# Noise values in the token rows, two weight halves moved, and a new order of output products in a two-layer mixture-of-experts kernel

## The reference

```python
# first mixture: 3072 x 8 logits, greedy from the largest, cap = 384 tokens per expert
logits = x @ w_gate
for e in range(E):
    h = np.maximum(x[assigned == e] @ w1[e], 0.0)
    out[assigned == e] = h @ w2[e]
# second mixture, on the first one's output
logits = x @ w_gate
noise_scale = np.log1p(np.exp(x @ w_noise))
noisy_logits = logits + noise_scale * noise        # noise: one row of 8 values per token
top2 = np.argpartition(-noisy_logits, 2, axis=1)[:, :2]
...                                                # softmax over the two, sum of both experts
```

## Time and profile before

| | us |
|---|---|
| median of 3 runs (1318.83 to 1322.05) | 1318.96 |
| profiled execution, device time | 1320.37 |
| its span, first to last instruction | 1318.5 |
| TensorE busy | 1231.4 (93%) |
| VectorE busy | 914.4 (69%) |
| ScalarE busy | 572.1 (43%) |
| GpSimd busy | 286.2 (22%) |

### The profile page before, as it was taken

How to read it: one execution, slowest core, us unless ns; L and a number is a source line. 1 busy time by engine, 2 the same in 40 slices (tenths; PEclk the granted TensorE clock), 3 DMA queues, 4 the chain that set the end, 5 groups by cost and what they waited for, 6 DMA issues and landing times.

```text
span 1318.5 us, 27799 instructions
## 1 busy us (share of the span) xinstructions
PE 1231.4 (93%) x9680; PEld 1096.5 (83%) x9680; DVE 914.4 (69%) x1818; ACT 572.1 (43%) x1224; POOL 286.2 (22%) x346
## 2 busy tenths in 40 slices
PE   7999983299999999999999999999999999999997
PEld 6888872278787787888898999989999898999986
DVE  4777765887887888765696666666666666766662
ACT  4666650123333233344415544544455444544541
POOL 4000000202202102120213323324233242333322
PEclk9999995589999999999999999999999999999999
DMA  7878744433332432543315233233333423334210
GB/s 146 169 169 163 166 97 182 153 113 109 125 120 70 147 133 65 194 147 107 110 34 192 72 107 111 81 104 106 126 123 120 144 79 104 100 125 135 88 43 13
DMA packets 174298, 154.65 MB, mean 117 GB/s; under 512 B 105117, under 2 KB 137885, under 8 KB 174240
## 3 DMA queue, kind: packets, MB, share of 16 engines
q1 hardware_dynamic: 151552, 102.83, 27.8%
q0 software_dynamic: 16128, 44.56, 11.0%
q10 hardware_dynamic: 6560, 6.49, 1.4%
HBM read 206.13 MB, written 33.75 MB: 182 GB/s over the span
## 4 chain that ended last, share of the span: by engine, by line
PE 38%; issue 37%; DVE 10%; POOL 9%; DMA 3%; ACT 1%; POOLq 1%; DVEq 0%; SPq 0%; ACTq 0%
PE bank L789 8%; PE bank L769 8%; DMA out<-result,token_now 3%; PE bank L645 3%; POOL partial L421 3%; POOL out L431 3%; PE bank L654 2%; PE bank L633 2%; POOL held L401 2%; PE bank L1001 2%; PE bank L669 2%; POOL x L405 2%; PE bank L715 2%; PE bank L1028 2%; PE bank L754 1%
## 5 line engine op out<-in xcount | busy, mean ns | idle before, releaser
L572 DVE TENSOR_TENSOR w_part<-w_sb,w_part 128x1024 fp32r<-128x1024 f32 x280 | 341.7, 1224 | 97.1 <-ACT w_part L566 89.1
L566 ACT CAST w_part<-w_sb 128x1024 fp32r<-128x1024 f32 x280 | 290.6, 1046 | 205.1 <-PE bank L1028 152.2
L1001 PEld LDWEIGHTS bank<-x2T,w_part 128*128 128x128 f32 x2688 | 326.3, 192 | 4.6 <-DVE x2T L1558 1.6
L1001 PE MATMUL bank<-x2T,w_part 128*128 128x256 f32 x2688 | 327.9, 283 | 1.8 <-DVE x2T L1558 1.8
L1028 PE MATMUL bank<-w_part,h2T 128*128 128x512 f32 x1344 | 312.6, 391 | 0.0
L1028 PEld LDWEIGHTS bank<-w_part,h2T 128*128 128x128 f32 x1344 | 250.2, 188 | 51.0
L789 PE MATMUL bank<-w_part,hT 128*128 128x512 f32 x576 | 156.5, 409 | 3.7 <-DVE w_part L572 3.7
L769 PE MATMUL bank<-xgT,w_part 128*128 128x384 f32 x768 | 146.5, 344 | 0.9 <-DVE xgT L1222 0.9
L1913 ACT ACTIVATE h2T<-bank 128x512 fp32r<-128x512 f32 x112 | 66.9, 598 | 180.4 <-PE bank L1001 141.3
L379 POOL DMA_INDIRECT xg<-x_dram,token_of x24 | 29.6, 1232 | 507.0 <-DVE token_of L1258 266.0
L769 PEld LDWEIGHTS bank<-xgT,w_part 128*128 128x128 f32 x768 | 133.6, 191 | 2.9 <-DVE xgT L1222 1.4
(11 more groups left out here) (281 smaller groups left out, 1306.2 us busy)
## 6 DMA issues: line engine op xcount, KB each, us to landing
w_sb<-in_moe_w SPq DMA_DIRECT2D x280, 512.0 KB
k_in<-in_k SPq DMA_DIRECT2D x32, 240.0 KB
v_in<-in_v SPq DMA_DIRECT2D x32, 240.0 KB
q_in<-in_q SPq DMA_DIRECT2D x32, 192.0 KB
x_dram<-x_sb SPq DMA_DIRECT2D x32, 192.0 KB, 3.1
out<-zeros SPq DMA_DIRECT2D x1, 6144.0 KB, 19.7
y_dram<-y_sb ACTq DMA_DIRECT2D x24, 256.0 KB, 2.0
x<-y_dram,slot_now POOLq DMA_INDIRECT x56
```

Of the source, the lines that this page charges most:

```text
L566: scalar.copy(split_part(0, c), raw_part(c)).then_inc(hi_ready[c], 1)
L572: nc.vector.tensor_tensor(split_part(1, c), raw_part(c), split_part(0, c).bitcast(F32), ALU.subtract).then_inc(lo_ready[c], 1)
L1001: last = nc.tensor.matmul(bank[2 + g % 2][:, at:at + TILE], w1_part[a][:, kt, f * P:(f + 1) * P], x2T[b][:, kt, :], start=(f % 2 == 0 and ...
```

## The change

Three things change.

1. `x_dram` gets rows of 520 values: 512 of x and the token's 8 noise values. ScalarE's queue issues one copy of the whole noise array into the last 8 columns, after the attention has stored x. The gather of a token row brings its noise along, and a new ScalarE instruction, `copy_noise`, copies it to `noise_g` behind `xg_high(k, 2)`. The 24 noise gathers go. GpSimd's first gather waits for the copy (`noise_stored`), the later ones for `copy_noise` of the expert before.
2. Low halves move in VectorE's `step`: w1's last quarter (c = 3) from digit 6 to digit 5, between `met` and `delta`; w2's first quarter (c = 4) from behind `chosen` to digit 6; w2's second (c = 5) from the end of the step to behind `chosen`. ScalarE's high halves of c = 4 and 5 move with them.
3. The 24 products are done in the order 0 to 5, 8, 9, 6, 7, 10 to 23, in all bodies, and `before_votes[2]` goes from 9 to 10.

```diff
@@ TensorE
+            order = tuple(range(6)) + (8, 9, 6, 7) + tuple(range(10, TPE * FT))
             def combine(e, a, b):
-                for i in range(a, b):
+                for i in order[a:b]:
...
-                before_votes = (0, 6, 9, 12, 15, 20, 22)
+                before_votes = (0, 6, 10, 12, 15, 20, 22)
@@ VectorE, step, per digit s
                         if s >= 3:
-                            w_low(k, s - 3, 1)
+                            w_low(k, s - 3 if s < 6 else CH, 1)
                     dve.wait_ge(counts_up, n * len(SHIFTS) + s + 1)
...
+                        if s == 5:
+                            w_low(k, 3, 1)
                         if s == 6:
                             xg_low(k, 1)
@@ VectorE, step, behind the digits
                     xg_low(k, 2)
-                    w_low(k, CH, 1)
+                    w_low(k, CH + 1, 1)
...
                 if k is not None:
-                    w_low(k, CH + 1, 1)
                     s1_low(k, 3)
@@ ScalarE, step
                     xg_high(k, 0)
+                    w_high(k, CH, 1)
...
                     xg_high(k, 2)
-                    w_high(k, CH, 1)
+                    copy_noise(k)
+                    w_high(k, CH + 1, 1)
...
                     s1_high(k, 0)
-                    w_high(k, CH + 1, 1)
                     s1_high(k, 1)
@@ ScalarE, new
+            def copy_noise(e):
+                nc.scalar.copy(noise_g[:, bass.ds(e * TPE, TPE), :], xg[:, :, DM:DM + E]).then_inc(noise_in, 1)
...
+            act.dma_start(x_dram[:, DM:DM + E], moe2_noise[:, :]).then_inc(noise_stored, 16)
@@ GpSimd
                     pool.wait_ge(xg_turned, e * TPE)
+                    pool.wait_ge(noise_in, e)
+                else:
+                    pool.wait_ge(noise_stored, 16)
...
-                for c in range(e * TPE, (e + 1) * TPE):
-                    pool.indirect_dma_start(out=noise_g[:, c, :], out_offset=None, in_=moe2_noise[:, :],
```

## The result

Eight runs of each kernel on the same chip gave 1323.49 us for the changed kernel (1322.73 to 1324.66) and 1319.56 for the kernel before: ratio 1.0027, 95% interval [1.0018, 1.0036]. The change costs 3.6 us by the ratio and 3.9 by the medians, where my sum had 2.1. The profiled execution took 1323.39 us with a span of 1321.6 (before 1320.37 and 1318.5).

A forecast was written before the change was run, and what follows sets the result against it. The prediction took the hand-overs between TensorE and VectorE in the expert loop as the bound. Its terms, 1.05 - 0.6 + 0.25 + 0.5 + 0.9 = +2.1 us, gave 1321.1 us on the median 1318.96; range 1314.9 to 1323.8.

The forecast's parts named there:

- Products 8 and 9 ahead: Five loop steps: TensorE's 0.76 us wait turns into other waits, each step ends 0.21 us later; +1.05 us.
- the three waits I named: TensorE's new waits in the loop: for `above` of digits 2 and 3 and for `met` of digit 3.
- The eighth step: Step of experts seven and eight: a later `copy_y` delays ScalarE's queue and TensorE's third transpose by 0.87 us; +0.9 us.
- ScalarE's copy: Loop: the new noise copy on ScalarE makes the low half, tally and tie flags 0.1 us later; +0.5 us.
- The low half at the end of the step: w2's second quarter leaves the place before the last `s1_low`: gain 0.12 us a step, -0.6 us over five.
- The inserted low half: w1's last quarter between `met` and `delta` of digit 5: cover suffices by 0.11 us; +0.25 us over five steps.
- The rival in which it is paid: The half inserted at digit 5 delays TensorE by 0.55 us a step, giving 1323.8 us; chance 0.10.
- The noise: Noise gathers leave GpSimd, one copy into token rows is through before the first gather: 0 us, bounds 0 and +1.
- The waits simply vanish: Rival: TensorE's 0.76 and 0.58 us waits per loop step are gained whole, 6.6 us, giving 1312.4; chance 0.12.
- half of them: Rival: the 0.24 us lead is kept and the 0.58 us gained, -4.1 us, giving 1314.9; chance 0.04.
- The noise gathers cause the odd wait: Rival: they cause VectorE's 2.06 us idle before `met` of digit 5; without them 0.25 us return, 1320.8; chance 0.09.
- The port rule: Skill's rule that two-SBUF-input VectorE and SBUF-reading GpSimd instructions block each other; low half would lose up to 1 us.

The follow-up runs named there:

- e2_order: The kernel before with only the new product order (8 and 9 ahead of 6 and 7): 1320.65 us, ratio 1.0011.
- e4_noise: The kernel before with all noise edits of the change, but the old product order and weight halves: 1322.23 us, ratio 1.0022.
- e1_pad96: The kernel before with rows of xg 96 bytes a partition wider, so the buffers behind it begin 96 bytes later: 1322.37 us, ratio 1.0020.
- e3_halves: The kernel before with only the moved weight halves, noise still gathered by GpSimd: 1319.92 us, ratio 1.0005.
- e12_fill_halves: e11_fill with the moved weight halves of the change added: 1313.90 us, ratio 0.9957 to the kernel before.
- e13_place96: The kernel before with xg's rows unchanged and 96 unused bytes a partition behind them, moving the later buffers: ratio 1.0018.
- e9_one_ahead: The kernel before with only product 8 ahead of 6 and 7 in the loop's steps and fillings redistributed: 1315.94 us, ratio 0.9971.
- e0_again: The kernel before, unchanged, run and profiled a second time: 1318.79 us, ratio 1.0000.
- e11_fill: The kernel before with loop fillings moved to TensorE's waits: product 0, products 8 and 9, and the last gate product earlier: 1314.25 us, ratio 0.9961.
- e8_pad64: The kernel before with 64 unused bytes a partition behind xg, moving the later buffers by 64 bytes: ratio 1.0017.

## Why the prediction was right, and where not

**Products 8 and 9 ahead (+1.05).** Right, place by place: e2_order has +0.22 a step against my 0.21. Of the three waits I named two are there, 0.47 us before the count of s2 (I said 0.6) and 0.43 for `met` of s3. The 0.1 to 0.2 us before the count of s3 don't show.

**The eighth step (+0.9).** Right: +0.96 in e2_order, and the chain `copy_y`, high half, low half, `xg_low`, third transpose is the one forecast.

**ScalarE's copy (+0.5).** Right, path and size: 0.10 us a step between e4_noise and e1_pad96, by way of the low half and the tie flags.

**The low half at the end of the step (-0.6).** Its size was wrong: 0.0 us in e3_halves. I had taken off what `s1_low` waits for ScalarE and kept 0.12 us, and had not followed it beyond the count of s0. In the changed kernel the count of s0 does come 0.18 us sooner, but from it to the vote of s1 it is 10.70 us instead of 10.48 (386.52 to 397.00): the next low half in VectorE's chain waits 0.22 us for ScalarE's high half, and that stands behind the hidden-layer matmuls, not behind the count.

**The inserted low half (+0.25).** 0.0 us in e3_halves and in the changed kernel. I had built it on `met` at 414.00. With `met` where the changed kernel has it, `delta` still waits 1.04 us for the vote and the half is hidden. So `above` of s6 ends 0.84 us ahead of the count (416.65 and 417.49), not within 0.2 as I had announced. Where `met` is late, as in e12_fill_halves, the half does cost some 0.16 us. The rival in which it is paid gave 1323.8, next to the median measured; for this profile it is wrong all the same, as that time has another cause.

**The noise (0, bounds 0 and +1).** This is the step that failed. GpSimd's gathers, the copy into the token rows and the wait for it cost nothing, as forecast: the copy of 96 KB, issued at 201.25, took 15.8 us and was through at 217, ahead of the first gather (the page's DMA issue, KB and us to landing, and GpSimd's timeline):

```profile
x_dram<-in_moe_noise ACTq DMA_DIRECT2D x1, 96.0 KB, 15.8
```

```profile
255.69 2.05 POOL L382 DMA_INDIRECT xg<-x_dram,token_of  x1 [238.25 <-issue]
```

That gather starts 2.1 us later than in the earlier trace rows; the first transpose of `xg` doesn't (260.28, before 260.5). But I had followed only the instructions of the edit, and not that a buffer grows and pushes others: by e13_place96 and e1_pad96 this costs 2.1 to 2.2 us in A and B, of which 1.6 are in the four periods and B, clear of the clock's return. It is also why the period is 51.73 and not the 51.4 to 51.5 that I had announced: 51.20 + 0.22 for the order + 0.10 for the copy is 51.52, and 0.22 for the place makes 51.74.

So the sum, with measured terms, is 1.0 + 1.0 + 0.5 + 0 + 0 + 2.2 = 4.7 us, near the 4.46 of A and B together (with 0.25 for the copy, as A and B have it, 4.45). By the medians it is 3.9, by the ratio 3.6. One thing lies on the other side: in both profiles of the kernel before the granted clock falls to 0.50 for 3.4 us between 637 and 642 us, with TensorE busy throughout before and after, and nine matmuls (three products) take 3.70 and 3.89 us there instead of 2.36. So it is not full everywhere outside 200 to 260 us, as I had written; it also stays at the lower level until some 273 us. The row of the second profile (PE, PEld, DVE, ACT, POOL busy, then PEclk) and that of the changed kernel:

```profile
638.00:642.00 4.00, 4.00 (x15) 3.18 (x14) 2.69 (x3) 0.71 (x2) 1.95 (x2) 0.62 0.23 71
```

```profile
638.00:642.00 4.00, 4.00 (x36) 3.42 (x34) 3.66 (x14) 1.84 (x3) 0.00 (x0) 1.00 0.33 60
```

A mean of 0.62 is a mixture of 2.4 GHz and the lower level of 1.2. It makes the kernel before 1.2 to 1.4 us longer (from the ranks of `owner` to the first transpose of `x` 20.0 and 20.2 us, in the changed kernel 18.9), which nearly closes the sum: 4.46 and 0.2 from the last transpose of `xg` to the ranks of `owner` (31.4 to 31.6 us) are 4.7; less 1.3 it is 3.4, by the spans 3.1. Whether the timed runs have it too, and why the changed kernel doesn't, isn't shown.

**The number.** 1323.49 us is inside the range by 0.3 us, and that is partly luck. The range reached up to 1323.8 only for the rival of the paid low half, which isn't what happened, and it held a loss of some 2 us for which I had no term. The sum of +2.1 is 1.5 to 1.8 us short of the measured 3.6 to 3.9. That is about what is left when the loss of some 2.2 us and the 0.35 that two terms without effect (-0.6 and +0.25) had taken off are set against the 1.2 to 1.4 us of the clock's fall in the kernel before, if the timed runs have it.

**The rivals.** The waits simply vanish, or half of them: fallen, by e2_order and e3_halves. Yet e9_one_ahead shows that 0.70 us of the 0.76 can be had; it is the fillings that decide, and two products at one place were one too many there. The noise gathers cause the odd wait: not alone, by e0_again; whether they have a part in it is open. The port rule of the Trainium skill (SBUF — State Buffer, Who interferes with whom) doesn't show in the loop: the low half of s5 takes 1.25 us beside a noise gather in the kernel before and 1.23 without one in the changed kernel. I had left out that the same section of the Trainium skill infers an exception for this pair: an instruction of VectorE like this one takes only the read side of the shared ports, and writing a DMA's descriptors needs the write side. The trace agrees with that.

## What to carry to other kernels

In this loop a wait on TensorE was gained only where the filling between two hand-overs ended just as VectorE was ready, and where the piece moved forward was left out later, at a place where VectorE waited for TensorE. Look for both before you move work forward. Filling that is taken out may have been hiding something. Before a buffer is made wider, ask which operands of matmuls lie behind it; measure the empty widening by itself. A single odd row of one execution is worth a second profile before anything is built on it, and worth looking for again in every later one.

## What was not expected of the hardware

Moving fp32r operands by 96 bytes within each partition makes 768 matmuls of 128x384 take 347 ns instead of 342 to 344 on average, 148.2 us instead of 146.2, and a step of 51.2 us 0.22 us longer; by 64 bytes 0.03, by 128 bytes 0.14. VectorE stood idle 2.0 us before the same instruction in five steps of one execution, and in no step of the next one of the same kernel; in four other kernels' profiles it did so again, and in e11_fill and e12_fill_halves TensorE lost 1.1 us a step by it. Between 280 us and the last matmuls the granted clock fell to 0.50 once, for 3.4 us, near 640 us in both profiles of one kernel, and of the others only in e8_pad64, for as long.
